# An attention recurrence by levels on one core: k kept in blocks of 32 tokens, the odd groups' outputs in the other head's rows, and a new order of work on three engines

## What is computed

```python
B, H, S, D = 4, 8, 768, 48
state = zeros((B, H, D, D))
for t in range(S):
    cur = einsum('bhd,bhe->bhde', u * k[t], v[t])
    y[t] = einsum('bhd,bhde->bhe', r[t], state + cur)
    state = w[t][..., None] * state + einsum('bhd,bhe->bhde', k[t], v[t])
```

## Time and profile before

| | us |
|---|---|
| median of 3 runs (lowest, highest) | 920.03 (918.13, 922.46) |
| the profiled execution | 915.25 |
| its span, first to last instruction | 913.5 |
| TensorE busy in it | 877.8 (96%) |
| VectorE busy | 487.1 (53%) |
| ScalarE busy | 390.3 (43%) |

### The profile page before, as it was taken

One profiled execution on the slowest core, in us unless ns is written; L12 is line 12 of the kernel. 1 busy time (PEld: TensorE's weight loads), 2 busy tenths in 40 slices (PEclk: granted clock), 3 DMA queues, 4 the chain that ended last, 5 costly groups with the idle time before them and its releaser, 6 DMA issues.

```text
span 913.5 us, 26366 instructions
## 1 busy us (share of the span) xinstructions
PE 877.8 (96%) x10791; PEld 802.4 (88%) x10792; DVE 487.1 (53%) x868; ACT 390.3 (43%) x725; POOL 155.8 (17%) x111
## 2 busy tenths in 40 slices
PE   5889999999989999999999999999999999999995
PEld 4789999997779999999999789899899899899895
DVE  7679999999754244334333670550640641631620
ACT  4467777777442243224323650540530620621510
POOL 1000000000283545254425101000001001001000
PEclk9899999999789999999999999999999999999998
DMA  7356666672174764565468410010010010000000
GB/s 292 118 179 245 241 242 241 244 258 77 31 237 132 168 164 81 182 165 162 77 190 186 83 36 27 9 34 26 9 43 17 9 43 26 0 9 26 1 17 18
DMA packets 45182, 99.21 MB, mean 109 GB/s; under 512 B 11904, under 2 KB 32032, under 8 KB 41184
## 3 DMA queue, kind: packets, MB, share of 16 engines
q1 hardware_dynamic: 40240, 86.02, 30.2%
q0 software_dynamic: 3936, 11.60, 4.5%
q10 hardware_dynamic: 976, 1.18, 0.4%
HBM read 83.84 MB, written 14.96 MB: 108 GB/s over the span
## 4 chain that ended last, share of the span: by engine, by line
PE 90%; DVE 3%; issue 2%; POOL 1%; ACT 0%; POOLq 0%; DVEq 0%; ACTq 0%
PE y_banks L1357 22%; PE h_banks L1347 22%; PE h_banks L1318 13%; PE y_banks L1331 12%; PE yt L320 5%; PE yt L342 4%; PE ms L354 3%; PE sc L262 3%; PE sc L257 2%; PE ms L282 2%; PE xt_ps L1299 1%; PE ms L294 1%; POOL W L1006 1%; PE sc L269 1%; PE sc L260 1%
## 5 line engine op out<-in xcount | busy, mean ns | idle before, releaser
L1357 PE MATMUL y_banks<-W,g 128*128 128x384 f32 x1152 | 200.8, 334 | 0.0
L1357 PEld LDWEIGHTS y_banks<-W,g 128*128 128x128 f32 x1152 | 200.0, 188 | 0.5
L1347 PE MATMUL h_banks<-yT,W 128*128 128x512 f32 x864 | 198.9, 392 | 0.8 <-POOL yT L1258 0.8
L1347 PEld LDWEIGHTS h_banks<-yT,W 128*128 128x128 f32 x864 | 162.1, 188 | 36.2 <-issue 1.2
L1422 ACT ACTIVATE relu<-h_banks 128x512 f32<-128x512 f32 x96 | 57.5, 599 | 235.0 <-PE h_banks L1347 235.0
L1318 PE MATMUL h_banks<-xT,W 128*128 128x448 f32 x576 | 119.7, 369 | 2.8 <-POOL W L1006 2.8
L1331 PE MATMUL y_banks<-h,W 128*128 128x448 f32 x576 | 120.9, 368 | 0.0
L1318 PEld LDWEIGHTS h_banks<-xT,W 128*128 128x128 f32 x576 | 109.4, 190 | 11.7 <-issue 3.0
L1331 PEld LDWEIGHTS y_banks<-h,W 128*128 128x128 f32 x576 | 107.0, 188 | 8.7
L1499 DVE TENSOR_TENSOR relu<-relu 128x512 f32<-128x512 f32 x96 | 66.5, 692 | 68.3 <-ACT g L1426 67.9
L1517 DVE COPY stage<-y_banks 128x384 f32<-128x384 f32 x24 | 13.4, 558 | 164.9 <-PE y_banks L1357 164.9
(11 more groups left out here) (171 smaller groups left out, 1016.9 us busy)
## 6 DMA issues: line engine op xcount, KB each, us to landing
stage<-in_w SPq DMA_DIRECT2D x16, 1536.0 KB, 7.6
V<-in_vs SPq DMA_DIRECT2D x16, 1296.0 KB, 7.9
RK<-in_rkw SPq DMA_DIRECT2D x15, 1160.0 KB, 5.2
y_columns<-y_sb SPq DMA_DIRECT2D x8, 672.0 KB, 3.6
x_rows<-xs SPq DMA_DIRECT2D x32, 144.0 KB, 6.9
yb<-y_columns SPq DMA_DIRECT2D x5, 768.0 KB, 4.4
stage<-in_w_in SPq DMA_DIRECT2D x2, 1536.0 KB, 9.7
stage<-in_w_out SPq DMA_DIRECT2D x2, 1536.0 KB, 10.8
```

The costliest lines, as they stand in the source:

```text
L1347: ins = pe.matmul(h_ps[f % BANKS][:], w_in_of[wp][:, f // NF1, k, f % NF1 * P:(f % NF1 + 1) * P], yT[yp][:, k, :], start=(k == 0 and i == ...
L1357: ins = pe.matmul(y_ps[s % 2][:, 0:X], g[gp][:, f, s * P:(s + 1) * P], w_out_of[wp][:, f, :], start=(f == 0 and i == 0), stop=(f == NF2 - ...
```

## The change

1. The orders in which k is kept at levels 1 to 4 (`KEPT`, `k_into_next`) now differ by rotations inside blocks of 32 tokens, not of 128; the move at level 1 takes two instructions on each of VectorE and ScalarE, and the move at level 4 reads every second word where it read every eighth.
2. The output rows of odd groups are those of the other head (`rows_of(h ^ g)`) in `within` and `from_states`. `from_states` is one pass in which head and group alternate. `turn` gets gate columns for either case, with the identity between them, and `copy_x` reads the turned rows accordingly.
3. The order of work in the bodies of TensorE, ScalarE and VectorE.

```diff
-TURN = P + 16
+GATED = 16
+TURN = GATED + P
-KEPT = ((0, 5, 6, 4, 3, 2, 1), (1, 0, 5, 6, 4, 3, 2), (2, 1, 0, 5, 6, 4, 3), (3, 2, 1, 0, 5, 6, 4), (5, 6, 4, 3, 2, 1, 0),
+KEPT = ((0, 5, 6, 4, 3, 2, 1), (5, 6, 1, 0, 4, 3, 2), (5, 6, 2, 1, 0, 4, 3), (5, 6, 3, 2, 1, 0, 4), (5, 6, 4, 3, 2, 1, 0),
         (6, 5, 4, 3, 2, 1, 0))
+KIN = 32
-    turn = [sb(f"turn{s}", [P, TURN]) for s in range(2)]
+    turn = [sb(f"turn{s}", [P, 2 * TURN]) for s in range(2)]
...
         if l == 1:
-            k = k.rearrange("p (g d x a) -> p g a d x", d=2, x=32, a=2)
-            new = new.rearrange("p (g a d x) -> p g a d x", a=2, d=2, x=32)
...
-        elif l == 4:
-            k = k.rearrange("p (g u y x) -> p g x y u", u=16, y=4, x=2)
-            new = new.rearrange("p (g y x u) -> p g x y u", y=4, x=2, u=16)
+            k = k.rearrange("p (g d y x c) -> p c d g y x", d=2, y=4, c=2, g=GROUPS)
+            new = new.rearrange("p (g y c d x) -> p c d g y x", d=2, y=4, c=2, g=GROUPS)
+            return [(new[:, side, d], k[:, side, d]) for d in range(2)]
+        elif l < LEVELS - 1:
+            k = k.rearrange("p (b x c) -> p b c x", b=S // KIN, c=2)
+            new = new.rearrange("p (b c x) -> p b c x", b=S // KIN, c=2)
...
-            sp.dma_start(turn[p.s][:, P:TURN], gates[bass.ds(p.index % DEEP, 1)].rearrange("o p x -> (o p) x")).then_inc(v_loaded[p.s], 16)
+            sp.dma_start(turn[p.s][:].rearrange("p (a x) -> p a x", a=2)[:, :, 0:GATED],
+                         gates[bass.ds(p.index % DEEP, 1)].rearrange("o p (a x) -> (o p) a x", a=2)).then_inc(v_loaded[p.s], 16)
...
-                            y = out[rows_of(h)]
+                            y = out[rows_of(h ^ g)]
...
-        def from_states(p, swapped):
+        def from_states(p):
...
                     for h in range(2):
-                        g = h ^ swapped
-                        i = 2 * c + g
-                        chunk = i * 2 + q
-                        if chunk:
-                            ins = pe.matmul(chunk_of(yt[rows_of(h), g * 512 + c * P:g * 512 + (c + 1) * P], q),
-                                            St[rows_of(h), :, chunk - 1], chunk_of(R2[p.s][rows_of(h), i * P:(i + 1) * P], q),
-                                            start=False, stop=bool(swapped), skip_group_check=True)
+                        for g in range(2):
+                            i = 2 * c + g
+                            chunk = i * 2 + q
+                            if chunk:
+                                ins = pe.matmul(chunk_of(yt[rows_of(h ^ g), g * 512 + c * P:g * 512 + (c + 1) * P], q),
+                                                St[rows_of(h), :, chunk - 1], chunk_of(R2[p.s][rows_of(h), i * P:(i + 1) * P], q),
+                                                start=False, stop=True, skip_group_check=True)
...
             chunk_states(z)
+            scores(y, 4)
             for l in range(2, LEVELS):
                 within(z, l)
-            scores(y, 4)
             scores(x, 1)
-            from_states(z, 0)
-            from_states(z, 1)
+            from_states(z)
+            scores(y, 5)
             scores(x, 2)
-            scores(y, 5)
             turn_y(z)
...
             move_k(y, 3)
+            spread_t(z, zz)
             copy_k_rows(z)
-            spread_t(z, zz)
             copy_kv(z, zz)
             move_k(x, 1)
             move_k(y, 4)
             copy_scores(y, 4)
-            move_k(y, 5)
             scale_r(x1)
             copy_yt(z, zz)
             move_r(x, z)
+            move_k(y, 5)
             copy_scores(y, 5)
...
             x, y, z = (pair(n, o - d) for d in range(3))
+            scale_k(y, 3)
+            scale_k(x, 0)
+            scale_r(y, 3)
             t_product(x, 0)
+            mask_scores(y, 3)
             scale_r(x, 0)
-            scale_k(x, 0)
-            scale_k(y, 3)
-            scale_r(y, 3)
             scale_k(x, 1)
-            mask_scores(y, 3)
             mask_scores(x, 0, z)
+            scale_r(y, 4)
             pass_states(z)
-            scale_r(y, 4)
             scale_k(y, 4)
             mask_scores(x, 1)
+            t_product(x, 1)
             scale_r(x, 1)
-            t_product(x, 1)
+            t_product(x, 2)
             scale_r(x, 2, z)
+            scale_k(y, 5)
+            t_product(x, 3)
             scale_k(x, 2)
-            t_product(x, 2)
+            t_product(x, 4)
             mask_scores(x, 2)
-            t_product(x, 3)
-            t_product(x, 4)
             t_product(x, 5, z)
-            scale_k(y, 5)
             scale_r(y, 5)
```

More of the change, by code:

```diff
@@ L126, in k_into_next @@
         if l == 1:
-            k = k.rearrange("p (g d x a) -> p g a d x", d=2, x=32, a=2)
-            new = new.rearrange("p (g a d x) -> p g a d x", a=2, d=2, x=32)
[L129 to L134, removed]
-        elif l == 4:
-            k = k.rearrange("p (g u y x) -> p g x y u", u=16, y=4, x=2)
-            new = new.rearrange("p (g y x u) -> p g x y u", y=4, x=2, u=16)
-        else:
-            k = k.rearrange("p (g y z x) -> p g y z x", y=2, z=2, x=32)
-            new = new.rearrange("p (g z y x) -> p g y z x", z=2, y=2, x=32)
-        return new[:, :, side], k[:, :, side]
+            k = k.rearrange("p (g d y x c) -> p c d g y x", d=2, y=4, c=2, g=GROUPS)
[4 more added lines that the diff above has]
+            new = new.rearrange("p (b c x) -> p b c x", b=S // KIN, c=2)
+        else:
+            k = k.rearrange("p (g y z x) -> p g y z x", y=2, z=2, x=KIN)
+            new = new.rearrange("p (g z y x) -> p g y z x", z=2, y=2, x=KIN)
+        return [(new[:, :, side], k[:, :, side])]
     def block_of(l):
@@ L325, in within @@
                 ins.then_inc(within_done[p.s], 1)
-        def from_states(p, swapped):
+        def from_states(p):
             if p is None:
                 return
[L330 to L334, removed]
+            pe.wait_ge(st_ready[p.s], p.twos + 1 + LEAD)
+            pe.wait_ge(within_done[p.s], p.twos + 1)
+            pe.sem_inc(carrier, 1)
             for c in range(CP):
@@ L337, in from_states @@
                     for h in range(2):
-                        g = h ^ swapped
-                        i = 2 * c + g
-                        chunk = i * 2 + q
-                        if chunk:
-                            ins = pe.matmul(chunk_of(yt[rows_of(h), g * 512 + c * P:g * 512 + (c + 1) * P], q),
-                                            St[rows_of(h), :, chunk - 1], chunk_of(R2[p.s][rows_of(h), i * P:(i + 1) * P], q),
-                                            start=False, stop=bool(swapped), skip_group_check=True)
-            if swapped:
-                ins.then_inc(y_full[p.s], 1)
+                        for g in range(2):
[5 more added lines that the diff above has]
+                                                start=False, stop=True, skip_group_check=True)
+            ins.then_inc(y_full[p.s], 1)
         def turn_y(p):
@@ L352, in turn_y @@
             for i in range(GROUPS):
-                at = i // 3 * 512 + i % 3 * TURN
-                ins = pe.matmul(ms[:, at:at + TURN], yT[:, i % 2, i // 2 * P:(i // 2 + 1) * P], turn[p.s][:], start=True, stop=True)
+                odd = i % 2
+                at = odd * 512 + i // 2 * TURN
+                ins = pe.matmul(ms[:, at:at + TURN], yT[:, odd, i // 2 * P:(i // 2 + 1) * P], turn[p.s][:, odd * GATED:odd * GATED + TURN],
+                                start=True, stop=True)
             ins.then_inc(xt_full[p.s], 1)
@@ L408, in _ @@
         for s in range(2):
-            act.dma_start(turn[s][:, 0:P], consts[:, MASK_COLS:MASK_COLS + P]).then_inc(turns_loaded, 16)
+            act.dma_start(turn[s][:, GATED:TURN], consts[:, MASK_COLS:MASK_COLS + P]).then_inc(turns_loaded, 16)
         def scale_r(p):
@@ L441, in move_k @@
             act.sem_inc(carrier, 1)
-            out, k = k_into_next(p, l, 1)
-            nc.scalar.copy(out, k).then_inc(k_moved[p.s][l], 1)
+            for out, k in k_into_next(p, l, 1):
+                ins = nc.scalar.copy(out, k)
+            ins.then_inc(k_moved[p.s][l], 1)
         def copy_yt(p, before):
@@ L504, in copy_x, with turned @@
             act.sem_inc(carrier, 1)
-            src = ms[:].rearrange("p (a y) -> p a y", a=2)[:, :, 0:3 * TURN].rearrange("p a (i t) -> p a i t", t=TURN)
-            out = xs[:].rearrange("p (a i) x -> p a i x", a=2)
+            out = xs[:].rearrange("p (i a) x -> p a i x", a=2)
+            def turned(even, odd, cols):
+                return bass.AP(ms, even, [[2 * 512, P], [512 + odd - even, 2], [TURN, CP], [1, cols]])
             for h in range(2):
                 cols = slice((p.s * 2 + h) * D, (p.s * 2 + h + 1) * D)
-                nc.scalar.copy(out[:, :, :, cols], src[:, :, :, rows_of(h)])
-            nc.scalar.copy(lgp[:, bass.ds(p.index * GROUPS, GROUPS), :].rearrange("p (a i) e -> p a i e", a=2),
-                           src[:, :, :, P:TURN]).then_inc(xs_ready[p.s], 1)
```

(23 more changed lines are left out.)

## The result

The changed kernel takes 910.0 us (median of 5 runs, 908.25 to 914.38) against 920.03: a ratio of 0.9894, with a 95% interval of 0.9863 to 0.9926. The forecast was 911.4.

The account below looks back on a forecast made before the run. TensorE and VectorE both fill the half step; VectorE then sets 11.53 - 0.42 - 0.29 + 0.07 = 10.89 us. Thirteen steps at 0.63 give 8.2, the last 0.4: 8.6 off 920.03, 911.4 us; own range 907 to 915.

Parts of the forecast that it names:

- Which engine bounds: Attention half step: both engines fill 11.53 us before; after the change VectorE sets it at 10.89, TensorE at 10.73.
- r times states: TensorE, from_states: 44 weight loads over four pieces take 1.1 us a half step instead of 2.35.
- The moves of k: VectorE: level 4 move from 0.84 to 0.55 or 0.56 us; level 1 in two pieces adds 0.07.
- Handovers: VectorE: waits where an instruction needs the one just before; new order removes all 0.42 us a half step.
- The later scan: VectorE's scan begins up to 0.46 us later behind scale_r(y, 4); TensorE's sum gets 0.45 us of wait.
- The copy of y: TensorE waits 0.42 us a half step ahead of the turns for ScalarE's copy; said to stay.
- the 0.9 us of TensorE waits: Sign named beforehand: TensorE waiting about 0.9 us a half step, half of it for the scan.
- TensorE's sum: TensorE's half step after the change: 11.53 - 2.35 + 1.1 + 0.45 = 10.73 us.
- The last step: Sixteenth attention half step (209.8 to 222.0 us): taken to gain 0.4 us.
- the slow first steps: First two attention half steps, one from 43.2 to 59.4 us: gain taken at nothing.
- The slow rival: from_states: loads stay shared, four pieces bring nothing; some 11.9 us a half step, 924 to 926 us; chance 0.22.
- The middle case: States' part takes 1.5 to 1.9 us, or an unseen wait 0.3 a step; 915 to 918 us; chance 0.18.

Follow-up runs that it names:

- e1: Kernel before with only the four pieces for r times states and the odd groups' swapped output rows; 925.17 us against 919.63, undisturbed half steps 11.54 us.
- e2: Kernel before with only the new orders of k (rotations within 32 tokens); 918.83 us, half step 11.57 us.
- e4: Kernel before with only the new order of work; 922.14 us, half step 11.76 us.
- e5: Changed kernel with r times states over two diagonal pieces at a time, loop over groups outermost; 918.52 us, half step 11.47 us.
- e8: Changed kernel with VectorE's products of decays back at their old places beside their users; 916.76 us, half step 11.37 us on average.
- e3: Kernel before with the new orders of k and the four pieces, in the old order of work; 915.18 us, half step 11.27 us.
- e7: Changed kernel with r times states over two pieces of one half of the partitions at a time, head outermost; 922.29 us, 11.64 us in most half steps.
- e11: Changed kernel with the scan ahead of scale_r(y, 4) on VectorE, as before the change; 913.34 us (ratio to before 0.9942), half step 11.16 us.
- e6: Changed kernel with two diagonal pieces at a time and adjacent words of St as weights (no longer computes the recurrence); 908.98 us, half step 10.94 us.
- e9: Changed kernel with all six products of decays of a pair on GpSimd; 911.36 us (ratio to before 0.992), half step 11.2 us.

## Why the prediction was right

- **Which engine bounds.** "VectorE sets the step, by little": 10.94 us measured, 10.89 by the sum. VectorE's own work is 10.86 of it, the rest the 0.08 ahead of scale_k(x, 0). That both engines held the old step with equal sums was the reading that mattered: e1 and e2 show that either saving alone is worth 0.03 us or nothing, e4 that the order alone costs 0.19; e5, e8 and e3 that undoing the four pieces, the places of the products of decays or the whole order loses 0.53, 0.43 and 0.33. The orders of k alone weren't undone in the changed kernel, so what they give there is not measured by itself.
- **r times states.** 1.1 us was taken for its loads and 1.32 measured, last load's length included; the pace per piece, 0.1 us a load, held with four pieces. The reason given for it, a load path per piece, fits e7 and the four pieces; a path shared by row group does not. A detail was misread: the text had the old passes on one diagonal and then the other, but both were on the same. It changed no number of the forecast, and made the expectation of e5 miss by 0.35 us.
- **The moves of k.** 0.84 to 0.53 us at level 4, 0.352 for each piece at level 1 as priced.
- **Handovers.** 0.42 us forecast. The gaps are gone from the timeline but for 0.05. That e8 loses 0.43 is close partly by chance, since it has another wait in every second step.
- **The later scan.** Costed as 0.45 us on TensorE and nothing on VectorE. On TensorE it was about 0.2 (e4); that VectorE would lose 0.22 without it (e11) was not in the sum. Since the sum took it in the new place anyway, it came out right.
- **The copy of y.** TensorE's 0.42 us of wait for it, said to stay, does so in e4 and e5. In the changed kernel TensorE waits 0.38 for scale_r(x, 1) instead, and the copy is done when the turns' place comes. Of the 0.9 us of TensorE waits that were to show it, half for the scan, only about 0.6 came, 0.2 for the scan.
- **TensorE's sum.** 10.73 us forecast, about 10.77 by e4 and e5 (9.45 + 1.32). That is luck in its parts: the states' part took 0.22 more than its 1.1, the later scan about 0.25 less than its 0.45. The step doesn't depend on it as long as it stays under VectorE's.
- **The whole.** 13 steps gave 7.2 us in the profiled execution, 8.2 by the sum: the first of them lay partly at half clock and took 11.74. The last step gave 0.1, not 0.4, and the slow first steps, taken at nothing, were 1.1 us longer. The difference of the medians is 10.0 us, with an interval of 6.8 to 12.6 that holds the forecast 8.6; the traces show only the 7.2 of it in the steps. So 911.4 lying 1.4 us from 910.0 is closer than the sum deserves. The mechanism is borne out by the half steps, not by that closeness.
- **The slow rival** was priced rightly, 11.9 a step against 11.76 in e4 for loads that gain nothing, but its condition, a shared load path, doesn't hold. The middle case didn't occur: RK lands after 5.2 us, and the waits of the changed kernel from 72.2 to 203.5 us name nobody who waits for it.

## What to carry over

Where two engines fill the same period, price each saving against the other engine's sum, and look for changes that have to come together. On an engine that sets the pace, count the places where an instruction needs the result of the one just before: each cost about 0.1 to 0.17 us here, and moving an independent instruction between them took nearly all of it away. Weights read at every twelfth word took 198 ns a load in e5, adjacent ones 120 in e6. Four array pieces instead of two made up for it (1.32 us for the 44 loads), and so did adjacent words over two pieces (1.14).

## What was not expected of the hardware

e1 saved TensorE work and yet lost time by the clock. Every step of e1 had 1.1 us of idle TensorE in one piece, and in four steps within 150 us the granted clock fell to 1.2 GHz for 3.4 us, 1.5 to 1.7 us of loss each; in its other steps it didn't. e3 had 0.9 us in one piece and no such fall in its steps, e7 only waits of 0.4 us and less ahead of a load and one fall. Each of them is one execution, so that the saving brought on the falls isn't shown, and what decides stays open.

GpSimd's float32 products slow VectorE's instructions that run beside them, from 0.56 us to as much as 1.09 (e9). With the waits that came with it, moving 1.2 us of work to an idle engine lengthened the step by 0.26 us.

Two passes over different pieces overlap at their seam even though each is paced by its loads: 1.99 us where 2.35 was taken (e5).
